# The first layer's second product as seven block products instead of eight

## The reference

```python
# 1: a linear attention with decay, 8 heads of 64
state = gamma * state + k_t v_t^T;  y_t = scale * q_t state
# 2: first layer, width 512 -> 1536 -> 512
xn = x / sqrt(mean(x*x) + 1e-6) * rms_g
g = xn @ w_gate;  out1 = (silu(g) * (xn @ w_val)) @ w_out
# 3: second layer, four experts, 512 -> 1024 -> 512, each weighted by p[:, e]
out += p[:, e] * (max(x @ w1[e], 0) @ w2[e])
```

## Time and profile before

| | us |
|---|---|
| runs (3) | 844.29, 844.63, 844.90 |
| median | 844.63 |
| profiled execution | 845.3 |
| its span | 843.5 |
| PE busy | 832.0 (99%) |
| DVE busy | 469.2 (56%) |
| ACT busy | 242.7 (29%) |
| POOL busy | 408.1 (48%) |

### The profile page before, as it was taken

One profiled execution on the slowest core, in us unless ns is written; L12 is line 12 of the kernel. 1 busy time (PEld: TensorE's weight loads), 2 busy tenths in 40 slices (PEclk: granted clock), 3 DMA queues, 4 the chain that ended last, 5 costly groups with the idle time before them and its releaser, 6 DMA issues.

```text
span 843.5 us, 12814 instructions
## 1 busy us (share of the span) xinstructions
PE 832.0 (99%) x4846; PEld 770.9 (91%) x4846; DVE 469.2 (56%) x776; ACT 242.7 (29%) x483; POOL 408.1 (48%) x460
## 2 busy tenths in 40 slices
PE   8999999999999999999999999999999999999998
PEld 7888999999999998889899989889899898898997
DVE  4698455545555558774554554545545545545545
ACT  2676222222322325422222222222212212222221
POOL 3998835546372739832836336336326325425100
PEclk9999999999999999999999999999999999999999
DMA  9801010100110010101101100110110110110003
GB/s 343 319 33 51 26 51 26 51 26 26 33 44 26 26 51 26 51 1 51 51 8 44 51 13 38 51 31 21 51 40 10 51 51 2 51 51 1 25 14 137
DMA packets 12876, 43.15 MB, mean 51 GB/s; under 512 B 1425, under 2 KB 1809, under 8 KB 12817
## 3 DMA queue, kind: packets, MB, share of 16 engines
q1 hardware_dynamic: 12528, 41.69, 14.0%
q10 hardware_dynamic: 288, 0.65, 0.2%
HBM read 39.19 MB, written 3.15 MB: 50 GB/s over the span
## 4 chain that ended last, share of the span: by engine, by line
PE 93%; POOL 2%; DMA 1%; DVE 1%; ACT 1%; issue 1%; SPq 0%; DVEq 0%
PE bank L520 30%; PE bank L521 30%; PE bank L522 30%; DMA ring<-qkv 1%; PE bank L469 1%; PE bank L462 1%; PE bank L449 1%; PE bank L499 1%; POOL w_lo L342 1%; POOL x_lo L237 0%; ACT x_hi L706 0%; DVE x_sum L233 0%; POOL wd_lo L361 0%; PE bank L482 0%; POOL squares L310 0%
## 5 line engine op out<-in xcount | busy, mean ns | idle before, releaser
L520 PE MATMUL bank<-x_hi,w_hi 128*128 128x384 f32 x784 | 263.9, 337 | 3.1 <-DVE x_lo L237 0.9
L522 PE MATMUL bank<-x_lo,w_hi 128*128 128x384 f32 x784 | 262.8, 335 | 0.0
L521 PE MATMUL bank<-x_hi,w_lo 128*128 128x384 f32 x784 | 262.8, 335 | 0.0
L1041 DVE SCALAR_TENSOR_TENSOR out_acc<-bank,p_norm,out_acc 128x512 f32<-128x512 f32 (+1 forms) x181 | 135.0, 746 | 127.7 <-PE bank L522 127.3
L520 PEld LDWEIGHTS bank<-x_hi,w_hi 128*128 128x128 f32 x784 | 147.2, 188 | 10.9 <-issue 5.5
L521 PEld LDWEIGHTS bank<-x_hi,w_lo 128*128 128x128 f32 x784 | 147.2, 188 | 5.5
L522 PE MATMUL bank<-wd_lo,h_hi 128*128 128x512 f32 (+1 forms) x386 | 152.0, 394 | 0.0
L521 PE MATMUL bank<-wd_hi,h_lo 128*128 128x512 f32 (+1 forms) x386 | 151.6, 393 | 0.0
L520 PE MATMUL bank<-wd_hi,h_hi 128*128 128x512 f32 (+1 forms) x386 | 149.9, 388 | 0.6 <-DVE out_acc L1037 0.3
L522 PEld LDWEIGHTS bank<-x_lo,w_hi 128*128 128x128 f32 x784 | 147.1, 188 | 0.0
L342 POOL TENSOR_TENSOR w_lo<-w_raw,w_hi 128x256 fp32r<-128x256 f32 x196 | 142.8, 762 | 3.0 <-ACT w_hi L678 0.8
(11 more groups left out here) (71 smaller groups left out, 874.5 us busy)
## 6 DMA issues: line engine op xcount, KB each, us to landing
w_raw<-wu SPq DMA_DIRECT2D x28, 512.0 KB, 4.3
ring<-qkv SPq DMA_DIRECT2D x23, 512.0 KB, 9.1
wd_raw<-wd SPq DMA_DIRECT2D x22, 512.0 KB, 3.5
out<-out_acc SPq DMA_DIRECT2D x11, 256.0 KB, 2.0
ring<-qkv ACTq DMA_DIRECT2D x1, 512.0 KB, 7.3
y_first<-t_y_decay SPq DMA_DIRECT2D x1, 256.0 KB, 8.0
out<-out_acc SPq DMA_DIRECT2D x2, 128.0 KB, 1.8
small_sb<-small ACTq DMA_DIRECT2D x1, 126.0 KB, 5.2
```

The costliest lines, as they stand in the source:

```text
L520: pe.matmul(dst, s_hi, m_hi, start=first, stop=False, skip_group_check=True)
L521: pe.matmul(dst, s_lo, m_hi, start=False, stop=False, skip_group_check=True)
L522: return pe.matmul(dst, s_hi, m_lo, start=False, stop=last, skip_group_check=True)
L1041: nc.vector.scalar_tensor_tensor(out=to, in0=new, scalar=p, in1=to, op0=ALU.mult, op1=ALU.add).then_inc(posted, 1)
```

## The change

The round's hidden operand is now a 2x2 block matrix too: rows are the token blocks (a), columns the two hidden blocks (v): A11 and A21 come from unit 2r, A12 and A22 from unit 2r+1. `w_out` gets block sums T1 to T4 as the first product's weights have. A round is seven block products (`DOWNS`), each in two tiles (the two 128-column halves s, banks 6 and 7) of three matmuls. M6, M7 and M4 go on in the bank in which M1 was, M3 in that of M5, and each of the 14 tiles is posted. `hidden` writes the raw blocks to SBUF; four sums (`hidden_sum`, DVE) are added; the high parts are made in four groups (one block A12; A11 and S2; S3 and A22; S1 and S4), and the low parts over the raw blocks in place, so the operand stands once. The tuples such as FIRST now give the number of tiles after each of the seven products. POOL's `split_wd` becomes four sums, one high part of seven blocks and seven low parts; for the first weights ACT makes the high part and DVE the low parts. To make room, buffers move and the reserved DMA scratch goes from its default to 2048 bytes. The waits of `product` for the banks of q-2 are on `hid_ready` in place of `h_ready`. Cut to its core:

```diff
+DOWNS = (("M2", "A12", "B21", True, ((0, 0),)), ("M1", "A11", "B11", True, ((0, 0),)),
+         ("M6", "S2", "T2", False, ((1, 0),)), ("M7", "S3", "T3", False, ((1, 1),)),
+         ("M4", "A22", "T4", False, ((0, 1),)), ("M5", "S1", "T1", True, ((1, 1),)),
+         ("M3", "S4", "B22", False, ((1, 0),)))
+
+HS = {"A12": 0, "A11": 1, "S2": 2, "S3": 3, "A22": 4, "S1": 5, "S4": 6}
+GROUPS = (slice(0, 1), slice(1, 3), slice(3, 5), slice(5, 7))
+GROUP_OF = {"A12": 0, "A11": 1, "S2": 1, "S3": 2, "A22": 2, "S1": 3, "S4": 3}
...
-FIRST, SECOND = (0, 1, 2), (2, 1, 2)
...
-END0, END1 = (0, 2, 2), (2, 1, 1)
-NEXT0, NEXT1 = (0, 1, 2, 2), (3, 0, 0, 0)
...
+FIRST, SECOND = (0, 0, 0, 2, 2, 2, 0), (0, 2, 2, 2, 2, 0, 0)
+EARLY, LATE = (0, 0, 0, 0, 2, 2, 2), (0, 2, 2, 2, 2, 0, 0)
+END0, END1 = (0, 0, 0, 2, 2, 2, 2), (2, 2, 0, 0, 2, 0, 0)
+NEXT0, NEXT1 = (0, 0, 0, 0, 2, 2, 2), (2, 2, 2, 2, 0, 0, 0)
+
+TILES, TILES_NEXT = (0, 1, 0, 1, 2, 0, 2), (0, 0, 0, 0, 2, 0, 4)
...
+            def wd_op(d, to, a, b):
+                i = d % 2
+                return nc.gpsimd.tensor_tensor(wd_raw[i][:, WS[to], :], wd_raw[i][:, WS[a], :], wd_raw[i][:, WS[b], :],
+                                               ALU.subtract).then_inc(wd_sums, 1)
+
+            def sum_wd_13(d):
+                pool.wait_ge(wd_in[d % 2], 16 * (d // 2 + 1))
+                wd_op(d, "T1", "B12", "B11")
+                wd_op(d, "T3", "B22", "B12")
+
+            def sum_wd_24(d):
+                pool.wait_ge(wd_sums, 4 * d + 1)
+                wd_op(d, "T2", "B22", "T1")
+                pool.wait_ge(wd_sums, 4 * d + 3)
+                wd_op(d, "T4", "B21", "T2")
+
+            def split_wd(d):
+
+                i = d % 2
+                sum_wd_13(d)
+                sum_wd_24(d)
+                pool.wait_ge(wd_sums, 4 * d + 4)
+                nc.gpsimd.tensor_scalar(wd_hi[i][:, :, :], wd_raw[i][:, 0:7, :], 1.0, 1.0,
+                                        ALU.mult, ALU.mult).then_inc(wd_hi_ready, 1)
+                pool.wait_ge(wd_hi_ready, d + 1)
+                for _, _, ws, _, _ in DOWNS:
+                    nc.gpsimd.tensor_tensor(wd_lo[i][:, WS[ws], :], wd_raw[i][:, WS[ws], :],
+                                            wd_hi[i][:, WS[ws], :].bitcast(F32), ALU.subtract).then_inc(wd_ready, 1)
...
-                    split_wd_lo(0)
+                    sum_wd_13(0)
                 elif n == 6:
+                    sum_wd_24(0)
                     part_lo(0, "A11")
...
                 if name == "M1" and 2 <= q < Q1 + 2:
-                    pe.wait_ge(h_ready, 2 * (q - 2) + 1)
+                    pe.wait_ge(hid_ready, 2 * (q - 2) + 1)
...
+            def down1(r, i):
+
+                n, p, s = T1N * r + i, r // J, i % 2
+                _, xs, ws, first, _ = DOWNS[i // 2]
+                pe.wait_ge(wd_ready, wd_count(p, i // 2))
+                pe.wait_ge(hid_split[GROUP_OF[xs]], r + 1)
                 if n == 0:
                     pe.wait_ge(x_normal, 16)
                 elif n >= 2:
                     pe.wait_ge(posted, n - 1)
-                for v in range(2):
-                    c, slot = slice(P * d, P * d + P), units[v] % SLOTS1
-                    mm = three(bank[6 + n % 2][:, 0:TB], wd_hi[p % 2][:, v, c], wd_lo[p % 2][:, v, c],
-                               h1_hi[:, slot, a, :], h1_lo[:, slot, a, :], v == 0, v == 1)
+                c = slice(P * s, P * s + P)
+                mm = three(bank[6 + s][:, 0:TB], wd_hi[p % 2][:, WS[ws], c], wd_lo[p % 2][:, WS[ws], c],
+                           h1_hi[:, HS[xs], :], h1_lo[:, HS[xs], :], first, True)
                 mm.then_inc(down_done, 1)
...
+            def unit(q, k=None, r=None, first=0, downs=(0,) * NP, tiles=(0,) * NP):
+
+
+                c, j = UNITS1[q] if q < Q1 else (F1 + UNITS2[q - Q1][0], UNITS2[q - Q1][1])
+                for place in range(NP):
+                    product(q, c, j, k, PRODUCTS[place][0])
+                    if q == 0 and place == 0:
+                        sum_squares(2)
+                    elif q == 0 and place == 2:
+                        sum_squares(3)
+                    for i in range(sum(downs[:place]), sum(downs[:place + 1])):
+                        down1(r, first + i)
                     for i in range(sum(tiles[:place]), sum(tiles[:place + 1])):
                         tile2(q - 1, i)
...
+            unit(0, 0)
+            unit(1)
+            unit(2, 1, 0, 0, EARLY)
+            unit(3, None, 0, sum(EARLY), LATE)
+            for r in range(1, F1 - 2):
+                unit(2 * r + 2, None, r, 0, FIRST)
+                unit(2 * r + 3, None, r, sum(FIRST), SECOND)
+            unit(Q1 - 2, None, F1 - 2, 0, END0)
+            unit(Q1 - 1, None, F1 - 2, sum(END0), END1)
+            unit(Q1, 2, F1 - 1, 0, NEXT0)
+            unit(Q1 + 1, None, F1 - 1, sum(NEXT0), NEXT1, TILES_NEXT)
...
-            def hidden_hi(q, a):
-                act.wait_ge(hid_ready, 2 * q + 2 - a)
-                nc.scalar.activation(h1_hi[:, q % SLOTS1, a, :], bank[3 * (q % 2) + 1 - a][:, 0:TB],
-                                     ACT.Copy).then_inc(hi_ready, 1)
+            def hidden_hi(r, g):
+
+                act.wait_ge(hid_sums, 4 * r + (2 if g == 2 else 4))
+                nc.scalar.activation(h1_hi[:, GROUPS[g], :], h1_raw[:, GROUPS[g], :], ACT.Copy).then_inc(hid_hi_ready[g], 1)
 
...
             def unit1(q):
 
+
+                r = q // 2 - 1
+                if q % 2 == 0:
+                    hidden_hi(r, 0)
+                    hidden_hi(r, 1)
                 copy_up(q, "M6", u2)
+                if q % 2 == 0:
+                    hidden_hi(r, 2)
                 silu(q, 0)
                 copy_up(q, "M7", u3)
+                if q % 2 == 0:
+                    hidden_hi(r, 3)
                 silu(q, 1)
-                hidden_hi(q, 1)
-                if q + 1 < Q1:
-                    copy_up(q + 1, "M1", m1)
-                hidden_hi(q, 0)
...
                     dve.wait_ge(c22_ready, q + 1)
-                    if q >= SLOTS1:
-                        dve.wait_ge(down_done, T1N * ((q - SLOTS1) // 2 + 1))
-                    x, y, to = c22[:, s, :], bank[3 * s][:, 0:TB], bank[3 * s][:, 0:TB]
+                    x, y = c22[:, s, :], bank[3 * s][:, 0:TB]
+                    to = h1_raw[:, HS["A22"], :] if v else h1_a21[:, :]
                 else:
                     dve.wait_ge(c12_ready, q + 1)
-                    x, y, to = bank[3 * s + 1][:, 0:TB], gate[:, s, :], bank[3 * s + 1][:, 0:TB]
+                    x, y = bank[3 * s + 1][:, 0:TB], gate[:, s, :]
+                    to = h1_raw[:, HS["A12" if v else "A11"], :]
                 nc.vector.tensor_tensor(to, x, y, ALU.mult).then_inc(hid_ready, 1)
...
+            def hidden_sum(r, to):
+
+                a21, a11, a12, a22 = (h1_a21[:, :] if n == "A21" else h1_raw[:, HS[n], :] for n in ("A21", "A11", "A12", "A22"))
+                s1, s2 = h1_raw[:, HS["S1"], :], h1_raw[:, HS["S2"], :]
+                x, y, op, of, count = {"S3": (a11, a21, ALU.subtract, hid_ready, 2), "S1": (a21, a22, ALU.add, hid_ready, 3),
+                                       "S2": (s1, a11, ALU.subtract, hid_sums, 2),
+                                       "S4": (a12, s2, ALU.subtract, hid_ready, 4)}[to]
+                dve.wait_ge(of, 4 * r + count)
+                if to == "S4":
+                    dve.wait_ge(hid_sums, 4 * r + 3)
+                nc.vector.tensor_tensor(h1_raw[:, HS[to], :], x, y, op).then_inc(hid_sums, 1)
+
+            def hidden_lo(r, g):
+                dve.wait_ge(hid_hi_ready[g], r + 1)
+                nc.vector.tensor_tensor(h1_lo[:, GROUPS[g], :], h1_raw[:, GROUPS[g], :],
+                                        h1_hi[:, GROUPS[g], :].bitcast(F32), ALU.subtract).then_inc(hid_split[g], 1)
...
+            def split_wd_lo_b(d):
+                dve.wait_ge(wd_hi_ready, d + 1)
+                nc.vector.tensor_tensor(wd_lo[d][:, 4:7, :], wd_raw[d][:, 4:7, :], wd_hi[d][:, 4:7, :].bitcast(F32),
+                                        ALU.subtract)
+
+            def split_wd_lo_t(d):
+                nc.vector.tensor_tensor(wd_lo[d][:, 0:4, :], wd_raw[d][:, 0:4, :], wd_hi[d][:, 0:4, :].bitcast(F32),
+                                        ALU.subtract).then_inc(wd_ready, NP)
...
+            def post1(r, first, last):
+
+                j = r % J
+                for i in range(first, last):
+                    n, s = T1N * r + i, i % 2
+                    name, _, _, _, ((half, a),) = DOWNS[i // 2]
+                    d = 2 * half + s
+                    dve.wait_ge(down_done, n + 1)
+                    to, new = x_all[j][:, d, a, :], bank[6 + s][:, 0:TB]
+                    if r < J and name not in ("M1", "M5", "M3"):
+                        nc.vector.tensor_copy(to, new).then_inc(posted, 1)
+                    else:
+                        dve.wait_ge(posted, n - 1)
```

(36 more changed lines are left out.)

359 lines of the change are left out of this document (160 added, 199 removed).

## The result

The changed kernel takes **872.21 us** (median of 4 runs, 871.69 to 873.27) against 844.76 of the kernel before on the same chip (4 runs): a ratio of 1.0326, 95% interval 1.0313 to 1.0339. It is slower, as forecast, but by 27.5 us where 11.1 were forecast, and above the range. (Of the runs further down, one of c5's four executions took 2094.57 us where the others took 851.63 to 852.76; nothing recorded explains it, and the table gives c5 without it.)

What follows compares the result with a forecast made beforehand. PE's queue of matmuls was taken as the bound. 845.3 + 6.8 (rounds 1 to 9) + 1.1 (start) + 3.2 (end) = 856.4, less 0.67: 855.7 us, 1.3% slower; range 840 to 866.

Steps and rivals of the forecast that it cites:

- PE's gain: Each round with its two units: 126 matmuls for 132, 1.04 us less, 12.5 for twelve rounds if PE never waits.
- The chain without POOL: Rounds with POOL quiet: a new serial chain makes PE wait 0.49 us before t4, t0's 0.31 inside it.
- What POOL adds: Rounds 1 to 9: POOL hinders DVE's chain, making the wait 2.6 us in odd rounds, 0.8 in even ones.
- Rounds 1 to 9: Five odd rounds at 2.6 and four even at 0.8 make 16.2 us, less 9.4 gained: +6.8.
- The start: Round 0: some 3 us of wait, 1.3 of old idle gone, 0.4 for t2 and t4, gain 1.04: +1.1.
- The end: Rounds 10 and 11, units 22 to 25: 8.7 us more DVE work against 4.0 free: +3.2 (-2 to +7).
- the cover holds: Rival: PE never waits, as A12's low part is done in time after M4's slot; 832.1 us, chance 0.10.
- POOL as a lock: Rival: each DVE instruction on the chain waits out one of POOL's, the high part in full; 865 us, chance 0.18.
- the last sign of being wrong: Whole kernel: steady rounds at 21.8 us and all loss at the edges would show the forecast wrong.
- theory B: Experiments' rival, no chance given: 14 posts, four sums, seven low parts a round overload DVE, or two banks are held too long.

Runs made afterwards that it cites:

- c5: Changed kernel with rounds' tiles one product later, early high parts, ACT's and DVE's queues reordered, the end's order, POOL's up-weight high part in seven pieces: 851.93 us.
- e4_later: Changed kernel with the first six tiles of rounds 1 to 9 one product later, DVE's posts following: 874.52 us.
- e3_high_early: Changed kernel with ACT's high parts of A12 and of A11 and S2 made as soon as their blocks are there: 869.87 us.
- e5_end_order: Changed kernel with two of DVE's posts in unit 25 moved ahead of and right behind the sum S4: 867.14 us.
- e8_quiet_end: Changed kernel with POOL's up-weight splits and operand low parts at the end cut to 2 columns, old low parts used: 862.05 us.
- e6: Changed kernel with round 0's first tiles placed later, behind unit 2's last and unit 3's first product, DVE's posts following: 872.95 us.
- c6: c5 with both edges rearranged (tiles later, copy of M7 ahead of hidden high parts, POOL's A12 before A22), pieces only for the first layer's weights: 853.45 us.
- c7: c6 with S4's high part ahead of the first hidden one, copy of M6 ahead of A12's high part, POOL's end work later: 856.15 us.
- c8: c7 with block 13's up weights split right behind the first operands' low parts, ahead of the down weights: 851.40 us.

## Why the prediction was right or wrong

*PE's gain*: right. 72 matmuls fewer, and 21.85-us rounds where nothing waits (c5, odd rounds).

*The chain without POOL*: right in place and nearly in size. 0.31 us before t0 forecast, 0.23 measured with POOL quiet; a quiet round 22.33 forecast (21.84 + 0.49), 22.38 to 22.41 measured. But it was one of two chains of nearly that length; the one through ACT's copy of M6 was given 0.4 us of room, and moving the tiles uncovered it.

*What POOL adds*: right in mechanism; even rounds 22.64 forecast, 22.51 measured; odd ones 24.44 forecast, 24.91 measured (24.72 without round 7 and its slow clock). 0.32 per instruction was taken; the means are 0.18 to 0.25 above free for the sums and 0.35 to 0.38 for the low parts. For the high part 0.8 was taken: in the round shown A12's low part ended 0.80 later than it would have. The choice of a value between "nothing" and 1.6 hid what matters: the hold is complete (e4_later's sum, e3_high_early's low part), and what it costs depends on when in POOL's 1.7 to 1.9 us the DVE instruction is issued. The Trainium skill, "SBUF — State Buffer", section "Who interferes with whom", has this rule, an exclusive lock for the whole instruction; this case's traces agree, 1.62 us for a sum of 0.56. The rival that took the rule at its word gave odd rounds of 25.9, too many, because it let four instructions on the chain wait 0.5 each and the high part be met at its very start.

*Rounds 1 to 9*: +6.8 forecast, +8.7 measured, 0.9 of it the clock in round 7, for which the sum had nothing.

*The start*, +1.1 forecast: **wrong**, +5.0. The wait before the first tile was to be some 3 us (the prediction's own times give 2.7 to 4.6), and it is 4.0; that part held, though DVE came to that low part at 83.9 instead of 83.2 at the latest. The two terms set against it failed: of the 2.1 us of old idle 1.3 were to go, and none did (PE is idle for 6.0 of 63.0 to 84.8 us, 4.0 more than the earlier trace rows, of which the long wait is 3.8); and nothing was set down for the clock behind a long wait, some 1.5 us (below).

*The end*, +3.2 forecast: **this is the step that failed most**, +13.0. It was reckoned as DVE's free time between 315.9 and 342.6 us against the durations added, "4.7 don't fit", less 1.5 that "the units behind give back". Free time in a stretch is not what matters when each post, sum and low part has its own date and stands in one queue. What the runs showed in its place: unit 25 loses 4.9 us by one wait, and the slow matmuls behind it, because a post stood in DVE's queue behind a low part and a sum (e5_end_order), and 8 us of the 13 go when most of POOL's work there is quiet (e8_quiet_end). The term had nothing for that, although and the earlier trace rows come from just this stretch, and nothing for the clock, which was at 1.2 GHz in two stretches of the end. No run has both edits, so how far the 4.9 and the 8 overlap is open; the wait that both touch fell by 1.0 in e8_quiet_end. That units 22 and 23 alone came out at +3.2 (26.65 for 23.43) is luck: the term was for units 22 to 25, and units 24 and 25 made the other 9.8.

*The rivals*: "the cover holds" fell at the point named for it. "POOL as a lock" was right about the lock and came nearest (865.6) for a reason that is not its own: its rounds were too long (a loss of 16.7 us in rounds 1 to 9 where 8.7 were measured) and its edges too cheap (4.3 where 18.0 were). Of the last sign of being wrong, "steady rounds at 21.8 us and all loss at the edges", the first half did not come, and two thirds of the loss is at the edges.

*Open*: how the start's loss is shared between DVE's load, POOL's and order. Three orders (e6, c6, c7) moved the wait from t0 to M4, then to M3 by way of POOL, and gained nothing that is clear of the scatter of U4; a quiet start was not tried. What stretched which instruction at the end is known in part only, since e8_quiet_end takes away POOL's instructions beside DVE's and POOL's own lateness in one. And theory B is out for the rounds only: of the kernels that do all the work none has an end under 64.16 us (c8), so a share of DVE's load in it isn't ruled out.

## What to carry to other kernels

A change that takes work off the bound engine and adds a serial chain must be priced wait by wait, with the order of every in-order queue that the chain passes, and the second-longest chain written down beside the first: moving one only shows the other. Free time of an engine over a stretch doesn't tell what its queue will make others wait: here 4.0 us were free, 3.2 of loss were forecast and 13.0 came. A DVE instruction with both inputs in SBUF is to be planned as held until the end of a long POOL instruction that reads SBUF (here to 0.4 or 0.8 us behind it), and long POOL instructions are to be put where no such DVE instruction is due, or cut into pieces if POOL has the time. Here the removal of work that brings 12.5 us on the bound engine was lost because it put this new kind of instruction on a chain and filled DVE's queue at the edges.
